# Score matmuls on 64 rows each, two heads in the two halves of the array, in an attention and two-layer MoE kernel

## What is computed

```python
scores = scale * np.matmul(q, k.transpose(0, 1, 3, 2))     # B=2, H=8, S=768, D=64
keep = is_sink | in_window       # the first 4 keys, and the 128 latest keys of each query
scores = np.where(keep, scores, -1000000000.0)
a = softmax(scores)
attn_out = np.matmul(a, v)
x = _moe_ref(x=attn_out rows, ...)      # layer 1, top 2 of 8
return _moe2_ref(x=x, ...)              # layer 2, top 1 of 8
```

## Time and profile before

| | |
|---|---|
| median of 3 runs | 752.75 us |
| span of the profiled execution | 750.6 us |
| busy TensorE, weight loads | 692.2 us (92%), 566.4 us (75%) |
| busy VectorE, ScalarE, GpSimd | 315.6, 288.0, 145.3 us |
| score matmuls L492, 192 records | 49.7 us busy, 385 ns mean |
| mean granted TensorE clock | 0.963 of full speed |

### The profile page before, as it was taken

One profiled execution on the slowest core, in us unless ns is written; L12 is line 12 of the kernel. 1 busy time (PEld: TensorE's weight loads), 2 busy tenths in 40 slices (PEclk: granted clock), 3 DMA queues, 4 the chain that ended last, 5 costly groups with the idle time before them and its releaser, 6 DMA issues.

```text
span 750.6 us, 14309 instructions
## 1 busy us (share of the span) xinstructions
PE 692.2 (92%) x3683; PEld 566.4 (75%) x3684; DVE 315.6 (42%) x610; ACT 288.0 (38%) x540; POOL 145.3 (19%) x210
## 2 busy tenths in 40 slices
PE   7999999189999999999999999997869999999993
PEld 6889898158888888888888888874637888788872
DVE  3565446665353524425435244221486512442211
ACT  5667667234343414325234143220335412341210
POOL 2400000031222222231312222201042211121101
PEclk9999999589999999999999999999869999999997
DMA  7788430625373634634516322214276711001100
GB/s 207 241 277 285 140 98 29 237 58 197 84 231 77 218 89 127 181 56 140 157 39 211 96 32 53 42 14 113 85 266 250 256 41 56 28 18 43 42 14 24
DMA packets 48865, 91.07 MB, mean 121 GB/s; under 512 B 5055, under 2 KB 11199, under 8 KB 48832
## 3 DMA queue, kind: packets, MB, share of 16 engines
q1 hardware_dynamic: 40320, 69.16, 27.4%
q0 software_dynamic: 8512, 21.50, 12.7%
HBM read 73.61 MB, written 17.56 MB: 121 GB/s over the span
## 4 chain that ended last, share of the span: by engine, by line
PE 85%; DVE 5%; DMA 3%; issue 2%; ACT 2%; SPq 1%; DVEq 0%; ACTq 0%; POOL 0%; POOLq 0%
PE banks L660 11%; PE banks L661 10%; PE banks L665 10%; PE banks L690 10%; PE banks L686 10%; PE banks L687 10%; PE banks L675 5%; PE banks L492 5%; PE banks L520 4%; PE banks L641 2%; PE banks L504 2%; PE banks L551 2%; DMA k_sb<-k_w 1%; DVE row_hot L1144 1%; PE banks L746 1%
## 5 line engine op out<-in xcount | busy, mean ns | idle before, releaser
L879 ACT ACTIVATE hTs<-banks 128x512 fp32r<-128x512 f32 x84 | 50.0, 597 | 313.1 <-PE banks L675 311.0
L660 PE MATMUL banks<-split,xTs 128*128 x336 | 136.5, 406 | 3.1 <-DVE split L988 2.3
L686 PE MATMUL banks<-split,hTs 128*128 x336 | 136.7, 407 | 1.3 <-ACT hTs L879 1.3
L661 PE MATMUL banks<-split,xTs 128*128 x336 | 132.8, 395 | 0.0
L687 PE MATMUL banks<-split,hTs 128*128 x336 | 132.8, 395 | 0.0
L1248 DVE TENSOR_TENSOR hTs<-banks,hTs 128x512 fp32r<-128x512 f32 x84 | 57.8, 690 | 163.8 <-ACT hTs L879 160.0
L988 DVE TENSOR_TENSOR split<-raw,split 128x2048 f32 (+1 forms) x44 | 99.3, 2289 | 52.7 <-ACT split L779 52.4
L690 PE MATMUL banks<-split,hTs 128*128 x336 | 92.4, 396 | 0.4 <-DVE hTs L1248 0.4
L779 ACT ACTIVATE split<-raw 128x2048 f32 (+1 forms) x44 | 82.3, 1907 | 25.9 <-issue 19.6
L665 PE MATMUL banks<-split,xTs 128*128 x336 | 91.8, 394 | 0.0
L443 POOL DMA_INDIRECT x_moe<-rows,dst x28 | 44.6, 1594 | 186.4 <-DVE rows L1256 184.6
(11 more groups left out here) (171 smaller groups left out, 743.9 us busy)
## 6 DMA issues: line engine op xcount, KB each, us to landing
raw<-w1a SPq DMA_DIRECT2D x16, 1024.0 KB
raw<-w2a SPq DMA_DIRECT2D x16, 1024.0 KB
k_sb<-k_w SPq DMA_DIRECT2D x12, 520.0 KB, 4.6
raw<-w1b SPq DMA_DIRECT2D x6, 1024.0 KB
raw<-w2b SPq DMA_DIRECT2D x6, 1024.0 KB
q_sb<-q_t SPq DMA_DIRECT2D x24, 128.0 KB, 3.5
x_attention<-rows SPq DMA_DIRECT2D x12, 256.0 KB, 4.7
split<-x_moe SPq DMA_DIRECT2D x12, 256.0 KB, 5.3
```

Of the source, the lines that this page charges most:

```text
L660: pe.matmul(psH[:, half, :], xTs[:, 0, c, :], weights(slot, 0, o), start=(c == 0), stop=False)
L661: pe.matmul(psH[:, half, :], xTs[:, 0, c, :], weights(slot, 1, o), start=False, stop=False)
L686: pe.matmul(psY, hTs[:, 0, c, :], weights(slot, 0, o), start=(c == 0), stop=False)
L879: act.activation(hTs[:, 0, half * 4:half * 4 + 4, :].rearrange("p c n -> p (c n)"), psHT[:, half, :], ACT.Copy).then_inc(s["h_high"], 1)
```

## The change

Each head's score matmul now reads only its own 64 partitions of q and of k: head 0 partitions 0 to 63, head 1 partitions 64 to 127. `q_sb` loses the axis of padded copies and is half as large, the two memsets and their semaphore go, and a unit's q is loaded by one DMA of 128 partitions, so that `qk_in[b]` rises by 32 per unit.

```diff
-            q_sb = early.enter_context(nc.sbuf_tensor("q_sb", [P, BATCH, PAIRS, 2, P], F32))
+            q_sb = early.enter_context(nc.sbuf_tensor("q_sb", [P, BATCH, PAIRS, P], F32))
...
-                q_unit = qT[bass.ds(i * BATCH + b, 1)].rearrange("a p j n -> (a p) j n")
-                for h in range(2):
-                    own = slice(h * HD, (h + 1) * HD)
-                    sp.dma_start(q_sb[own, b, :, h, :], q_unit[own]).then_inc(qk_in[b], 16)
+                sp.dma_start(q_sb[:, b], qT[bass.ds(i * BATCH + b, 1)].rearrange("a p j n -> (a p) j n")).then_inc(qk_in[b], 16)
                 sp.dma_start(k_sb[:, b], kW[bass.ds(i * BATCH + b, 1)].rearrange("a p j n -> (a p) j n")).then_inc(qk_in[b], 16)
...
                 if pair == 0:
-                    pe.wait_ge(qk_in[b], i * 48 + 48)
+                    pe.wait_ge(qk_in[b], i * 32 + 32)
...
                 for h in range(2):
-                    mm = pe.matmul(S[:, j % 2, h, 0:n], q_sb[:, b, pair, h, :], k_sb[:, b, pair, 0:n], start=True, stop=True)
+                    own = slice(h * HD, (h + 1) * HD)
+                    mm = pe.matmul(S[:, j % 2, h, 0:n], q_sb[own, b, pair, :], k_sb[own, b, pair, 0:n], start=True, stop=True)
                 mm.then_inc(scores_ready, 1)
...
-            pe.wait_ge(q_zeroed, 2)
...
-            for h in range(2):
-                dve.memset(q_sb[(1 - h) * HD:(2 - h) * HD, :, :, h, :], 0.0).then_inc(q_zeroed, 1)
```

More of the change, by code:

```diff
@@ L198, in build @@
         zero_ready = sem("zero_ready"); zeroed = sem("zeroed")
-        small_in = sem("small_in"); q_zeroed = sem("q_zeroed")
+        small_in = sem("small_in");
         v_early = [sem(f"v_early{b}") for b in range(BATCH)]; ones_ready = sem("ones_ready"); v_late = sem("v_late"); vs_in = sem("vs_in"); vs_masked = sem("vs_masked"); vs_parted = sem("vs_parted")
```

## The result

The changed kernel takes 759.21 us (median of five executions, from 758.08) against 752.75 us (752.30 to 755.01), a ratio of 1.0071 with a 95% interval of 1.0045 to 1.0097: slower by 0.7%. The forecast was 760.0 us. Two of the five executions took 775.78 and 785.91 us at a lower mean clock (0.936 and 0.921 against 0.964 to 0.966), where none of 65 executions of the kernel before took more than 756.44; the ratios, here and in the table of experiments, leave such executions out and the medians have them in, so that 0.7% is the cost without them. The profiled execution spans 756.3 us, 5.7 more than the 750.6 of before.

The account below looks back on a forecast made before the run. It took TensorE's chain through the attention as the bound, with shifts reaching the end one for one. Sum: 3.1+2.6+1.4+(1.55-0.7-0.7) = 7.25 us, 757.9 on the profiled span, 760.0 us as median; range 750.5 to 767.

Parts of the forecast that it names:

- A2 and B1: Head A's second and head B's first score pass, the only two said to overlap; 0.11 us saved per pair, bounds 0 and 0.22.
- A1 A2 B1 B2: Issue order of a pair's four score records on TensorE: two passes of head A, then two of head B.
- full-overlap rival: Score matmuls: the two middle passes overlap fully, saving 0.22 per pair, drains as priced; +3.3, 756.0 us; chance 0.22.
- The drains: TensorE empties at each shape switch: entry to the scores costs 0.11 to 0.20 us, exit to the transposes 0.21.
- +0.78: Net loss per loop unit of four pairs, in us, after overlap, drains and waits; unit of 11.8 us instead of 11.0.
- Four units +3.1: Attention's loop: four units at 0.78 us each lose 3.1 us.
- 20 to 62.6 us +2.6: Attention between 20 and 62.6 us: 14 pairs, priced by what precedes their scores, lose 2.6 us.
- last block +1.4: Last attention block, 106.7 to 131.1 us: six priced pairs lose 1.4 us, the last pair counted at nothing.
- Loads: Start of the kernel: one q DMA per unit lets k_sb be issued earlier; 0.7 us gained, bounds 0 and 1.3.
- The memsets: Two 0.9 us memsets on VectorE, hidden under the wait for k_sb: removal saves 0, without that cover 1.8 us.
- the forecast is wrong if a loop unit gets shorter: Refuting sign in the attention loop: the forecast has a unit grow from 11.0 to 11.8 us.
- 0.97 us from scores to transposes: Sign: first score to first transpose near 0.97 us with half overlap, 0.86 with full, 1.08 with none; 0.87 before.

Follow-up runs that it names:

- e12: Changed kernel with VectorE's router constants computed after block 1 and 14 instead of 7 warm-up matmuls: 747.67 us, ratio 0.9914.
- e3: Changed kernel with only block 0's score matmuls back to 128 rows, the two heads' scores summed there: 768.37 us, ratio 1.0218.
- e8: Changed kernel with one 128-row score matmul per pair in place of two of 64 rows, heads summed: 745.88 us, ratio 0.9925; only the attention counts.
- e11: Changed kernel with VectorE's router constants computed after block 1 instead of before it: 753.89 us, ratio 1.0002.
- e9: Kernel before, padded q and its loads kept, with only the scores of blocks 3, 4 and 5 reading 64 partitions: 748.93 us, ratio 0.9964.
- e13: Kernel before with the router constants computed after block 1 and 14 warm-up matmuls, the control: 750.38 us, ratio 0.9965.
- e1: Changed kernel with 14 instead of 7 warm-up matmuls: 772.96 us, ratio 1.0280.
- e4: Changed kernel with 14 warm-up matmuls and both heads' scores reading partitions 0 to 63: 856.09 us, ratio 1.1384; only the attention counts.
- e2: Kernel before with 14 instead of 7 warm-up matmuls, the control: 752.03 us, ratio 0.9995.
- e5: Changed kernel with the scores of two pairs issued together in every second step, half as many shape switches: 765.67 us, ratio 1.0092.
- e6: Changed kernel with the scores of two pairs issued together in every second step and 14 warm-up matmuls: 760.62 us, ratio 1.0138.
- e7: Kernel before with one small 64-row, 8-column matmul added ahead of each pair's scores, to price the switches: 766.46 us, ratio 1.0199.

## Why the prediction was right, and where it was not

**The overlap was mis-sized, and this turned the sign of the main term.** I let only A2 and B1 run together, since A1 A2 B1 B2 are issued in this order, and counted 0.11 us (0.22 in the full-overlap rival). The records show A1 with B1 and A2 with B2. Half of the stream goes: 2 x 0.22 = 0.44. My reason, that a load starts as the matmul before it starts, held for loads into the same rows only. The Trainium skill (TensorE: Matmul & The Clock Gate, Part 3), which I had weighed and given a chance of 0.22, was right: 7 ns apart here where it says some 4. The rival built on it also let only two of four passes meet.

**The drains were right in their place, to 0.01 us, both ways, and nearly so in their price.** Per unit, by starts of consecutive groups: the four score intervals fall from 0.96, 0.93, 0.87 and 0.88 to 0.64 each, -1.08; the groups ahead of the scores grow by 0.08 to 0.10, +0.36; the transposes behind them by 0.05 to 0.11, +0.27; the waits change by -0.10. Sum -0.55. The forecast was +0.78, and the difference, 1.33, is about four times 0.33, the missing overlap (0.44 - 0.11). Term by term: four times 0.44 saved is 1.76, and without the waits -0.45 was measured, so the eight switches of a unit cost 1.31 us, 0.33 per pair, where 0.65 at the entries and 0.84 at the exits, 1.49, had been forecast. The waits ate 0.10 and not 0.27. These two errors, 0.18 and 0.17, cancel; that is luck. With the right overlap the forecast of the loop would have come out as a number.

**Four units +3.1, 20 to 62.6 us +2.6, last block +1.4:** instead about -0.55 per unit from pair 13 on, -4.7 until pair 47. Block 0 at full clock costs 0.07 per step (1.19 in e12, 1.12 before), not 0.35: with two records of 0.11 saved, 0.22, its two switches cost 0.29, and the overlap that I had put at nothing there pays most of them.

**Loads:** k_sb lands earlier, the first scores start 1.48 us earlier; I had taken 0.7 and bounds of 0 and 1.3. Nobody waits for k_sb of b=1 any more. The memsets were hidden, as said. What I did not ask is what VectorE and GpSimd do at the same time when the one moves against the other.

**The clock was not in the forecast.** +10.5 us by pair 13 come from half clock up to 39.2 us and from the wait of 2.96 us. Shown by the runs: the 64-row matmuls of block 0 delay the first full clock (e3 and e8, one profiled execution each), the constants in VectorE's queue, 4.3 us longer beside the selects, make the wait (e11, e12: gone when the constants move), and with both removed the halves pay (e12, e9).

The start of pair 13 splits the 10.5: in e11, without the wait, it is at 37.64, 7.4 us late, with the half clock as the only large cause left, and the other 3.1 go with the constants. How much the two are worth at the end is known only roughly. By the ratios moving the constants brings 0.7% (after to e11) and the longer warm-up then 0.9% (e11 to e12); by the last transposes of rows of the profiled executions (136.88, 134.31, 124.48) it is 2.6 and 9.8 us. Their sum, some 12 us, agrees. Nor is all of the first part the collision: moving the constants also takes their 2.2 us without a collision out of VectorE's queue, and in the kernel before, where the constants did not collide, both edits together brought 0.35% (e13). The two causes do not add up freely: with an early clock alone TensorE comes to the rows sooner and waits longer, 4.90 us, although the constants take 5.5 us there and not 6.5 (e1).

**Right for the wrong reason, by luck.** A loss of 10.5 us that I had not seen and a gain of 4.7 where I had put a loss of some 7 make +5.7; I had said +7.3. Of the signs that I had named one caught it, "the forecast is wrong if a loop unit gets shorter": it did. Another, 0.97 us from scores to transposes, read 0.64.

**Open:** what keeps the clock at half while 64-row matmuls run. The half stretches last 23.9 (e1), 41.0 (e3) and, with one half alone, the rest of the attention (e4), against 3.4 (e2) and 13.7 (e8) without 64-row matmuls. Fewer switches in e5 and e6 go with shorter ones (6.8 to 13.7), and e7, with switches and hardly any 64-row work, rose late but never fell, not even behind a wait of 1.85 us. The runs don't separate the drained time from the rows left unused. Nor was e4 or e8 run with the constants moved, and no run has the kernel after with the old order of the loads.

## What to carry over

Two matmuls in separate halves of the array overlapped pass by pass here although the kernel names one head's matmul whole before the other's, and the change from 128 to 64 rows and back cost about 0.3 us per pair: the gain is half of the stream less the two switches, so the stream must be long enough (256 and 260 columns pay, 0.44 saved; 128 don't quite, 0.22 saved). Do it where TensorE is already at full clock (from block 3 on it paid without any other edit, e9), and look at what a shift of one engine against another makes collide: here VectorE's constants with GpSimd's selects. A total that agrees with a forecast proves little; compare where, group by group, the time was gained and lost.

## Not expected of the hardware

- With all score matmuls in one half of the array the clock stayed half for the rest of the attention although TensorE was busy throughout (e4, granted clock 0.50 from 61.14 to 82.53 us with TensorE busy 21.39 of 21.39 us; one profiled execution, the other had the same mean clock, 0.85):

```profile
61.14:82.53 21.39, 21.39 (x78) 17.34 (x78) 6.50 (x21) 8.93 (x24) 0.45 (x1) 0.50 0.14 52
```

- After a wait of TensorE's of 1.8 us the kernel before lost the clock for 3.4 us (e2); after 4.9 us the kernel with halves lost it for 23.9 us (e1).
- VectorE's two-input operations of 32 and 96 columns, 0.19 to 0.26 us, took 1.07 to 1.18 us each beside GpSimd's selects of 1.14.
